# Moving on-chip tiles of a fused attention, experts and MLP kernel to multiples of 128 bytes

## The reference

```python
# 1: attention with a hash mask; B=2, H=8, S=768, D=64, 6 projection columns
q_bits, k_bits = (q @ proj > 0), (k @ proj > 0)
scores = q @ k.T / sqrt(D); scores = where(q_bucket == k_bucket, scores, -1e9)
x = softmax(scores) @ v            # then reshaped to 1536 tokens x 512
# 2: mixture of experts, each token to its best of 8; d=512, f=1024
expert_idx = argmax(x @ w_gate); gate_w = softmax(x @ w_gate)[expert_idx]
x[mask_e] = gate_w * (relu(x[mask_e] @ w1[e]) @ w2[e])
# 3: last layer; 512 -> 2048 -> 512
h = x @ w_in; out = where(h > 0, h, exp(min(h, 0)) - 1) @ w_out
```

## Time and profile before

| | |
|---|---|
| median of 3 runs | 810.99 us (810.89 to 811.6) |
| the profiled execution: time, and span of its instructions | 810.57 us, 808.9 us |
| mean granted clock of TensorE in it | 0.988 of full speed |
| busy: PE, PEld, VectorE, ScalarE, GpSimd | 95%, 82%, 52%, 42%, 45% |
| share of PE in the chain of work that ended last | 81% |

### The profile page before, as it was taken

One profiled execution on the slowest core, in us unless ns is written; L12 is line 12 of the kernel. 1 busy time (PEld: TensorE's weight loads), 2 busy tenths in 40 slices (PEclk: granted clock), 3 DMA queues, 4 the chain that ended last, 5 costly groups with the idle time before them and its releaser, 6 DMA issues.

```text
span 808.9 us, 13956 instructions
## 1 busy us (share of the span) xinstructions
PE 771.7 (95%) x4117; PEld 662.0 (82%) x4118; DVE 418.9 (52%) x768; ACT 343.1 (42%) x688; POOL 360.4 (45%) x459
## 2 busy tenths in 40 slices
PE   5899999999999749999999999999999999999996
PEld 4799999989999637888888888888888888888885
DVE  5888888888888674212212222244433443343332
ACT  4877877787778534212122222222222322222221
POOL 3334443444335253999999999339000100010001
PEclk9999999999999959999999999999999999999999
DMA  6476484445544368666676766512000100010001
GB/s 157 120 207 173 118 213 119 111 121 132 145 118 147 133 188 246 208 204 196 195 206 192 251 193 186 183 53 92 13 14 14 52 1 1 1 52 1 1 0 53
DMA packets 73303, 97.24 MB, mean 120 GB/s; under 512 B 33264, under 2 KB 36080, under 8 KB 73264
## 3 DMA queue, kind: packets, MB, share of 16 engines
q1 hardware_dynamic: 62560, 76.37, 33.9%
q10 hardware_dynamic: 8544, 13.27, 5.0%
q0 software_dynamic: 2160, 7.09, 2.4%
HBM read 59.57 MB, written 19.44 MB: 98 GB/s over the span
## 4 chain that ended last, share of the span: by engine, by line
PE 81%; DMA 5%; DVE 4%; issue 3%; SPq 2%; ACT 2%; POOL 1%; DVEq 0%; POOLq 0%; ACTq 0%
PE ps_s L700 14%; PE ps_s L702 14%; PE ps_s L701 14%; PE ps_t L794 5%; PE ps_t L795 5%; PE ps_t L793 5%; PE ps_t L637 4%; DMA key_lo_mask<-query_lo_hi 3%; PE ps_s L622 3%; PE ps_s L623 2%; PE ps_o L653 2%; PE ps_o L654 2%; PE ps_p L602 2%; PE ps_t L729 2%; DMA query_lo_hi<-query_hi_mask 2%
## 5 line engine op out<-in xcount | busy, mean ns | idle before, releaser
L577 POOL DMA_INDIRECT out_dram<-out_sb,token_of x12 | 11.6, 969 | 229.0 <-ACT out_sb L955 226.3
L883 ACT ACTIVATE probs<-ps_s,stats 128x768 f32<-128x768 f32 x96 | 95.4, 994 | 42.1 <-POOL stats L471 41.5
L1066 DVE TENSOR_REDUCE stats<-ps_s 128x1 f32<-128x768 f32 x96 | 91.5, 953 | 17.8 <-PE ps_s L623 17.4
L1079 DVE TENSOR_TENSOR pt_lo<-ps_t,pt_hi 128x384 fp32r<-128x384 f32 x192 | 96.9, 546 | 6.3 <-ACT pt_hi L874 6.1
L874 ACT ACTIVATE pt_hi<-ps_t 128x384 fp32r<-128x384 f32 x192 | 83.6, 489 | 13.3 <-PE ps_t L637 12.7
L469 POOL TENSOR_SCALAR stats<-stats 128x1 f32<-128x1 f32 x96 | 21.1, 220 | 138.5 <-DVE stats L1066 138.4
L637 PE MATMUL ps_t<-ident,probs 128*128 128x128 f32 x576 | 79.8, 274 | 1.3 <-DVE pt_lo L1079 1.2
L964 ACT ACTIVATE elu_e<-elu_e 128x512 f32<-128x512 f32 x48 | 30.4, 633 | 112.9 <-DVE elu_e L1290 107.9
L522 POOL TENSOR_TENSOR w_lo<-stage,w_hi 128x1024 fp32r<-128x1024 f32 x32 | 77.5, 2422 | 0.0
L522 POOL TENSOR_TENSOR w_lo<-late_stage,w_hi 128x1024 fp32r<-128x1024 f32 x32 | 77.0, 2423 | 0.0
L700 PE MATMUL ps_s<-w_hi,gT_hi 128*128 128x512 f32 x192 | 75.6, 394 | 0.0
(11 more groups left out here) (183 smaller groups left out, 1680.8 us busy)
## 6 DMA issues: line engine op xcount, KB each, us to landing
stage<-in_moe_w_dram SPq DMA_DIRECT2D x72, 256.0 KB, 3.2
late_stage<-in_moe_w_dram SPq DMA_DIRECT2D x56, 256.0 KB, 3.3
key_hi_hi<-query_hi_mask SPq DMA_DIRECT2D x30, 192.0 KB, 3.8
x_slots<-x_rows SPq DMA_DIRECT2D x19, 257.0 KB, 4.8
y_dense<-y_sb ACTq DMA_DIRECT2D x19, 256.5 KB, 3.8
xg<-x_slots ACTq DMA_DIRECT2D x16, 257.0 KB, 4.0
raw_qk<-in_q_dram SPq DMA_DIRECT2D x16, 192.0 KB, 3.2
raw_v<-in_v_dram SPq DMA_DIRECT2D x16, 192.0 KB, 2.8
```

What stands on the lines that cost most here:

```text
L883: a(probs[:, s % 4].rearrange("p (h c) -> p h c", h=2), ps_s[:, 2 * (s % 2):2 * (s % 2) + 2, 0:HW], ACT.Exp, bias=stats[:, 2, c], scale=st ...
L1066: v_.tensor_reduce(stats[:, 0, c], ps_s[:, 2 * (s % 2):2 * (s % 2) + 2, 0:HW], AX.XY, ALU.max).then_inc(max_found, 1)
L1079: v_.tensor_tensor(pt_lo[gb][where], ps_t[:, half, 0:HW].rearrange("p (t c) -> p t c", c=P), pt_hi[gb][where].bitcast(F32), ALU.subtract). ...
```

## The change

Only offsets change. `base` is rounded up to 128 instead of 32; `keep_end`, `xgT_hi`, the first `yT` tile and `elu_e` begin at the next multiple of 128; the floor under `x_rows` is raised by 128. No instruction is added, removed or moved on any engine.

```diff
-        base = (nc.sbuf_base + 31) // 32 * 32
+        base = (nc.sbuf_base + 127) // 128 * 128
+        def line(offset):
+            return (offset + 127) // 128 * 128
-        keep_end = c
+        keep_end = c = line(c)
-        x_rows, c = place("x_rows", [P, TT, XC], F32, max(c, keep_end + 37 * 1024 + 32))
+        x_rows, c = place("x_rows", [P, TT, XC], F32, max(c, keep_end + 37 * 1024 + 160))
-        xgT_hi, c = place("xgT_hi", [P, 2, KD, P], F32R, c)
+        xgT_hi, c = place("xgT_hi", [P, 2, KD, P], F32R, line(c))
-        yT_hi, yT_lo = [], []
+        yT_hi, yT_lo, c = [], [], line(c)
-        elu_e, o3 = place("elu_e", [P, BW], F32, keep_end)
+        elu_e, o3 = place("elu_e", [P, BW], F32, line(keep_end))
```

## The result

The changed kernel is slower: 815.3 us against 811.8 (medians of 12 runs each), a ratio of 1.0036 with a 95% interval of 1.0024 to 1.0049. The forecast was 807.6, worked out from the median of the first three runs, 811.0; the twelve are 0.8 above it, and that explains little of a miss of 7.7. Its profiled execution took 815.45 us, with a span of 813.7 against 808.9.

The account below looks back on a forecast made before the run. PE's streaming was taken as the bound. Gains of 1.5 us (second block) and 1.9 (experts) took 810.57 to 807.2; with 0.4 for the median, 807.6 us, range 806.8 to 808.6, 8 in 10 within 805.5 to 810.4.

Parts of the forecast that it names:

- The bound and the view: Whole kernel: PE, busy for 95% of the span, bounds it; the timeline's distance between matmul starts is the view.
- The 10 and 12 beats: DMA: a 256-byte piece starting 128 past a multiple of 256 should need 12 beats, one 64 past 10; priced 0.
- The 16-byte lines: SBUF lines of 16 bytes would make a start at 64 as good as 128: sum 0, time 811.0.
- the first reading: Second block's `inner`: a moving operand at 64 modulo 128 costs 6.7 ns more per matmul of 512 columns.
- the terms of the second block: Last layer, second block: aligned turned rows save 1.28 us in `inner` and 0.24 in `outer` behind, together 1.5 us.
- Rival 4: First and third block: `yT_hi0`, `yT_lo0` at 0 modulo 256 slow `inner`, losing 3.0 us against 1.5; 812.5 us; chance 0.05.
- the register: Experts' matmuls: the weights' address from a register causes their excess, so only the second block gains; 809.5 us; chance 0.25.
- The term of 1.9 us: Experts' matmuls: gain if the stationary start at 64 is the cause, the middle of 2.2 and 1.5 us.
- the excess behind a turn: Aligned `outer` takes 2.83 us just behind a turn; assumed for the experts' 24 matmuls, it gives 5.55 us, 0.08 gained per tile.
- Attention: Attention's matmuls and transposes: gain between 0 and 1.5 us, taken as 0; its end to stay within 0.5 us.
- The reading on `v_split`: Attention's values: `v_split`, stationary at 64, shows no cost, 172 ns against 173 for the aligned scores behind.

## Why the prediction was wrong

**The bound and the view: right.** PE's spacing in the timeline decided everything; the writes of ScalarE, VectorE and GpSimd moved by a few ns (597 and 599 for L918, 2422 and 2415 for L522 on `stage`), `raw_qk` lands in 3.2 us as before. The 10 and 12 beats that the prediction worked out from the Trainium skill's page "DMA: Bandwidth & Descriptors", section "How a descriptor splits into AXI transactions", didn't show in the landing of `raw_qk`. The 16-byte lines of the Trainium skill's page "SBUF — State Buffer", section "SBUF: two separate sides", don't account for a distance of 32 that costs 0.08 us per 12 matmuls.

**The step that failed** is the first reading: "a moving operand at 64 costs 6.7 ns more per matmul of 512 columns". The 6.7 ns were right, and so were the terms of the second block made of them, 1.5 us: moved alone it gains 1.48. But I took the cost for a property of one tile's start, where it belongs to a pair. The kernel before offered one tile at 64 among others at 128, which can't tell these apart. So in the forecast the second block's gain came without a word on the tiles that the change pushes *away* from the weights: `yT_hi0`, `yT_lo0` and `gT`, all still multiples of 128. With the distance rule the same table of addresses gives the loss. `inner` and `outer` of two blocks go from 2.72 to about 2.80, and `outer` of the second from 2.74; the second's `inner`, matched at last, stays at 2.76 behind it. Taken one at a time, `yT` costs 2.7 us and `gT` 3.8, and the second block saves 1.5: 5.0, where all together cost 4.6. Less the experts' 0.9 (below) that is 3.7, and the medians differ by 3.5.

**Rival 4** named the place and half of the price: it put `inner` of the first and third block at 2.80, with a chance of 0.05. Moved alone, these tiles cost 2.7 us where the rival said 3.0. It left out `gT`, the stationary operand, which made `outer` slow in all three blocks; that is why the second block gained nothing and the last layer lost 4.6 us, not the 3.0 of the rival less the 1.5. Its reason, that no row showed a moving operand at 0 modulo 256, was the right thing to be afraid of, though it too was a rule of single starts, which the kernel with all tiles 128 bytes higher refutes; its chance was too small for a class without a single row.

**The experts: cause half right, size half.** The placement was the cause and the register was not: the spacing settled at 227 ns. But again it was a distance, +64, and not the stationary start by itself. The term of 1.9 us measured 0.9 us. `hidden` went from 5.585 to 5.558 and `expert_out` from 5.598 to 5.578 (medians of the sums of 24 spacings), 0.047 us a tile, and 19 tiles make 0.9. That is a sum of spacings: the stretch from the first expert matmul to the first of `inner`, 233.34 us before and 233.72 after, doesn't show it. I had assumed the excess behind a turn that `outer` shows; behind a turn of `hid` it lasts, after the change, for 6 gaps in `hidden` and 10 in `expert_out`.

**Attention: nothing in sum, as forecast.** It ended 0.2 us earlier, and in the other kernels, whose attention is laid out as before or as after, between 0.7 us earlier and 2.1 us later: no gain can be read from that. The transposes of `probs` stand 109 ns apart before and after (medians), though their distance went from +64 to 0. The reading on `v_split` was short-sighted: its own spacings were no longer than the aligned ones, but the four scores behind them were. The four took 716 ns before and 696 after, the six of the values 1125 and 1130 (medians of 60). The kernels with the old placement of attention have 704 to 718 for the four and 1826 to 1847 for all ten, the two with the new one 696 and 1828: the scores gained, and whether the ten did isn't shown.

**The rest of the span.** The early expert tiles (the first 35 us) took 0.5 us longer after, of which PE waited 1.0 us more for `xgT_lo` (2.7 against 1.7 in all). That stretch varies between executions whatever the layout: in the kernel before and the eight experiments that alter only the last layer's tiles, the first expert matmul starts between 295.2 and 297.8 us, and the first of `inner` between 529.0 and 532.6, with 233.3 to 236.6 us from the one to the other. So it is not put down to the change.

## What to carry to other kernels

Judge the placement of matmul operands in pairs: here TensorE streamed at its best rate, 227 ns per 512 columns, when the moving and the stationary operand began in the same class modulo 256 bytes, and a multiple of 128 in itself gave nothing. This was seen with float32r matmuls that stream 512 columns; where 384 columns or transposes stream, in attention, little or nothing of it was seen. When a change moves many tiles, list for each matmul both starts before and after, the ones that are merely shifted along too; for the changed kernel one pad of 128 bytes mended it, and 809.19 against 812.39 is nearly the gain that had been forecast. That is in part luck, since the terms were 1.5 and 1.9 us and measured 1.5 and 0.9. And when a profile offers one odd case among like ones, ask what else that case differs in, here a distance as much as a start.

## What the runs showed that was not expected

- A mismatch costs 6 to 8 ns per float32r matmul of 128x512, 3% of its 227 ns, at a distance of 32 bytes already, and 2.4 ns at +64 once the spacing has settled.
- The effect outlives the mismatch: matched matmuls behind a run at 128 settle after three (`outer` behind `inner`, 2.74 us per 12) to seven (`inner` behind `outer`, 2.76) instead of taking 2.72. (Behind the one off matmul of three in the first `inner` above there is no such trail.) Which reading disturbs which, the streaming of the moving operand or the load of the next stationary one beside it, the runs leave open; nothing here took the two apart.
- With the same program ahead of it the last layer began up to 3.5 us earlier or later, while its own blocks repeat to 0.02 us (92.25 and 92.26 for the third, 89.44 to 89.48 for the first, where all is matched). An effect of a few us in this kernel is better read by stretch than from a single time.
